# Expert logits computed as eight extra columns of a matrix product, and what has to be prepared for that earlier

## The chip, the cores and the metric

The kernel runs on one core of one Trainium2 chip. The metric is the device time of one execution in microseconds (us), the median of several runs. The core's engines run side by side and synchronise by semaphores: TensorE (PE, with its weight loads PEld), VectorE (DVE), ScalarE (ACT), GpSimd (POOL) and the DMA queue of SyncE (SP).

## The reference

```python
# 1. attention: r, k, v are (4, 8, 768, 48); a decayed state per head
for t in range(S):
    cur = einsum('bhd,bhe->bhde', u[None] * kt, vt)
    y[:, :, t] = einsum('bhd,bhde->bhe', rt, state + cur)
    state = w[None, :, :, None] * state + einsum('bhd,bhe->bhde', kt, vt)
x = y.transpose(0, 2, 1, 3).reshape(3072, 384)
# 2. feed-forward, d_ff = 2048
h = x @ w_in
g = h - np.tanh(h)
x2 = g @ w_out                      # (3072, 384)
# 3. eight experts, one for each token (d_ff = 1024)
xn = x2 / (norm(x2) + 1e-6); en = expert_emb / (norm(expert_emb) + 1e-6)
logits = xn @ en.T / tau            # (3072, 8)
expert = argmax(logits); gate = softmax(logits)[expert]
out = gate * (maximum(x2 @ w1[expert], 0) @ w2[expert])
```

## The kernel before

The kernel has three stages, each a block with its own program for every engine. A block ends when all engines have ended theirs.

**Attention** goes over `CH` = 6 chunks of 128 time steps, and in each over `B` = 4 batches: 24 tiles, numbered `n = B * c + b`. For a tile SP loads about 1.2 MB into one of four sets of buffers, once the tile four places earlier is done (`summed`, counted by PE's last transposes of a tile, L525, and two other semaphores). POOL multiplies r by k (L290) and by u (L292), ACT sums the product over each head in eight pieces (L339, the "bonus"), and POOL multiplies v by these sums (`bv`, L301). DVE scales r and k two tiles ahead (`rs` L376, `ks` L377, and k once more as `kst`, L384, for the state), masks the scores (`am`, L442), adds up the result (L433) and advances the state (`state_sum` L457, `state` L461). PE computes scores (L489), the state's update (L502), the product with the state (L509), the masked scores by v (L517), and the transposes of `bv` (L525). The first and the last chunk are written out by the program, the four between are a loop. A piece of 128x512 of the weights `w_in` (b = 0, 1) and `w_out` (b = 2, 3) comes with each tile. ACT rounds it to the high part (L332), POOL forms the low part (L295): all the feed-forward's products are made of three, high by high, high by low and low by high. After its last tile PE runs eight rounds of `keep_warm` (products of the identity by itself, two records each, L76).

**The feed-forward** takes 6 groups `g` of 512 tokens, and in each 16 blocks `f` of 128 hidden units. For a block PE makes 9 products of 512 columns (`first`), ACT `usq`, `tanh` and `quad`, DVE `diff`, `poly`, `large`, a second step of `poly` and a predicated copy (which count `h_used` and `g_done`), ACT the high part `g_h` and DVE the low part `g_l` of the result. `second(g, f)` multiplies it by `w_out`: 12 products of 384 columns, three for each of four tiles of 128 tokens, in four banks `y_ps`. It comes `LAG` = 3 blocks after `first`. `SPLIT` = blocks 9, 11 and 13 also hold the split of the next group's x (ACT, then DVE, L901). In each block one piece of the experts' weights is loaded by SP, split by ACT (L827) and POOL (L705) and stored again as `w12_h` and `w12_l`: 96 pieces in 96 blocks. POOL's split waits for `g_done` of its block.

For the logits PE turns each finished tile of 128 tokens (`turn_x2`, three transposes, L750) and multiplies it by the normed embeddings (`logit`, three products of eight columns, two records each, L758); ACT copies the turned tile between. Five groups do this within the next group's blocks (`TURN`), the last one at the end. There the order on ACT is four copies of `y_ps` and four sums of squares (`square_sum`, L840).

**The experts' stage** sorts tokens by expert and computes 31 tiles.

## Time and profile before

| | us |
|---|---|
| median of 3 runs (lowest, highest) | 932.28 (931.85, 932.81) |
| the profiled execution's own time | 932.17 |
| its span in the profile | 930.1 |
| granted TensorE clock, mean over the span | 0.98 |

The profile shows one execution. Busy times of engines overlap; a row of the timeline gives start, duration, engine, line and operands, and in brackets how long the engine had been idle and what ended that. Line numbers are those of the program above. A granted clock of 1.00 is 2.4 GHz, of 0.50 1.2 GHz.

### The profile page before, as it was taken

To read this page: it belongs to the slowest core of one execution; us is meant where nothing else is said; L and a number is where in the kernel's file an instruction comes from. 1 tells how busy PE (TensorE), PEld (TensorE's weight loads), DVE (VectorE), ACT (ScalarE), POOL (GpSimd) and SP (SyncE) were. 2 spreads that over 40 slices of the span, in tenths; PEclk is the share of its full clock that TensorE was granted. 3 is DMA by queue.
4 is the path that set the end of the run, shared out by engine and by line. 5 is a ranking of instruction groups with operands and counts; after the bars stand their busy time and mean duration, and the time that the engine had idled before them with its cause. 6 is when DMAs were issued, how large, how long until landed. Compare 5 with 4: busy or idle time off the path is not lost. (4 is left out here: it accounts for less than half of the span.)

```text
span 930.1 us, 18916 instructions
## 1 busy us (share of the span) xinstructions
PE 876.5 (94%) x5314; PEld 788.3 (85%) x5315; DVE 606.2 (65%) x991; ACT 477.4 (51%) x1225; POOL 349.1 (38%) x372
## 2 busy tenths in 40 slices
PE   4887778999999999999999999889999999999995
PEld 4776667799998998999999999879989999898994
DVE  8899998899889889889989988641121211212110
ACT  3455555677766766766767765313233333333331
POOL 9789995233323323323223322232222232222211
PEclk8899999999999999999999999889999999999998
DMA  7799885665755855755755654678857836811100
GB/s 223 193 256 258 249 249 138 198 201 185 262 168 185 256 169 175 259 175 170 249 174 183 209 181 158 242 257 297 317 210 266 304 110 241 311 40 34 47 6 1
DMA packets 106810, 181.46 MB, mean 195 GB/s; under 512 B 11051, under 2 KB 32717, under 8 KB 106768
## 3 DMA queue, kind: packets, MB, share of 16 engines
q1 hardware_dynamic: 92816, 165.40, 54.8%
q0 software_dynamic: 3968, 10.82, 3.5%
q10 hardware_dynamic: 9984, 4.72, 1.9%
q8 instruction: 21, 0.34, 0.2%
q14 instruction: 21, 0.17, 0.1%
HBM read 116.41 MB, written 65.86 MB: 196 GB/s over the span
## 5 line engine op out<-in xcount | busy, mean ns | idle before, releaser
L705 POOL TENSOR_TENSOR ew_l<-ew_raw,ew_h 128x512 fp32r<-128x512 f32 x96 | 128.2, 1335 | 299.9 <-DVE poly L927 297.0
L649 PE MATMUL y_ps<-wout_h,g_h 128*128 128x384 f32 x384 | 129.5, 337 | 1.1 <-DVE g_l L918 1.1
L651 PE MATMUL y_ps<-wout_h,g_l 128*128 128x384 f32 x384 | 129.3, 337 | 0.0
L650 PE MATMUL y_ps<-wout_l,g_h 128*128 128x384 f32 x384 | 129.1, 336 | 0.0
L1346 DVE TENSOR_TENSOR ex_hT_l<-e_bank,ex_hT_h 128x512 fp32r<-128x512 f32 x62 | 39.9, 686 | 127.4 <-ACT ex_hT_h L1496 127.4
L649 PE MATMUL h_ps<-xT_h,win_h 128*128 (+1 forms) x288 | 115.8, 402 | 2.1 <-DVE diff L908 2.1
L808 ACT ACTIVATE usq<-h_ps 128x512 f32<-128x512 f32 x96 | 55.9, 582 | 115.7 <-PE h_ps L651 102.9
L651 PE MATMUL h_ps<-xT_h,win_l 128*128 (+1 forms) x288 | 113.5, 394 | 0.0
L650 PE MATMUL h_ps<-xT_l,win_h 128*128 (+1 forms) x288 | 113.4, 394 | 0.0
L1373 POOL DMA_INDIRECT out_dram<-ex_o_sb,put_i x31 | 31.1, 1003 | 210.0 <-ACT ex_o_sb L1480 192.6
L1496 ACT ACTIVATE ex_hT_h<-e_bank 128x512 fp32r<-128x512 f32 x62 | 33.7, 596 | 122.3 <-PE e_bank L1406 118.2
L1338 DVE TENSOR_TENSOR ex_xT_l<-e_bank,ex_xT_h 128x384 fp32r<-128x384 f32 x31 | 17.3, 558 | 116.9 <-ACT ex_xT_h L1472 106.4
L1404 PE MATMUL e_bank<-w_h,ex_hT_h 128*128 x248 | 86.6, 349 | 1.3 <-ACT ex_o_sb L1480 1.3
L1406 PE MATMUL e_bank<-w_h,ex_hT_l 128*128 x248 | 84.1, 339 | 0.0
L1405 PE MATMUL e_bank<-w_l,ex_hT_h 128*128 x248 | 83.8, 338 | 0.0
L908 DVE TENSOR_TENSOR diff<-h_ps,tanh 128x512 f32<-128x512 f32 x96 | 66.1, 688 | 25.9 <-ACT tanh L809 25.4
L927 DVE COPY_PREDICATED poly<-large,diff 128x512 f32<-128x512 uint8 x96 | 71.7, 747 | 16.8 <-DVE poly L923 16.8
L1488 ACT ACTIVATE ex_hid<-e_bank 128x512 f32<-128x512 f32 x62 | 37.2, 599 | 79.5 <-PE e_bank L1406 79.5
L1404 PE MATMUL e_bank<-w_h,ex_xT_h 128*128 x186 | 76.0, 409 | 1.2 <-DVE ex_xT_l L1338 1.2
L649 PEld LDWEIGHTS y_ps<-wout_h,g_h 128*128 128x128 f32 x384 | 72.1, 188 | 5.7 <-issue 1.4
L650 PEld LDWEIGHTS y_ps<-wout_l,g_h 128*128 128x128 f32 x384 | 72.2, 188 | 4.2
L339 ACT ACTIVATE rku_out<-rku 128x48 f32<-128x48 f32 x192 | 43.7, 229 | 60.1 <-POOL rku L292 60.1
(206 smaller groups left out, 2126.2 us busy)
## 6 DMA issues: line engine op xcount, KB each, us to landing
ew_raw<-in_w SPq DMA_DIRECT2D x96, 256.0 KB, 3.1
w_h<-ew_h SPq DMA_DIRECT2D x96, 256.0 KB, 3.2
w_l<-ew_l SPq DMA_DIRECT2D x96, 256.0 KB, 2.0
w_h<-w_h SPq DMA_DIRECT2D x16, 1536.0 KB
w_l<-w_l SPq DMA_DIRECT2D x16, 1536.0 KB
rT_sb<-in_rT SPq DMA_DIRECT2D x48, 96.0 KB, 2.6
kT_sb<-in_kT SPq DMA_DIRECT2D x48, 96.0 KB, 2.8
k_sb<-in_k SPq DMA_DIRECT2D x24, 192.0 KB, 3.0
```

The costliest lines, as they stand in the source:

```text
L339: last_sum = act.activation(rku_out[:, head], rku[:, b % 2, head], ACT.Copy, accum_out=bonus[:, b % 2, h:h + 1])
L649: pe.matmul(out, lh, rh, start=start, stop=False)
L650: pe.matmul(out, lh, rl, start=False, stop=False)
L651: return pe.matmul(out, ll, rh, start=False, stop=stop)
L705: pool.tensor_tensor(ew_l[:, s, :], ew_raw[:, f % SPARE, :], ew_h[:, s, :].bitcast(F32), ALU.subtract).then_inc(ew_l_made, 1)
L808: act.activation(usq[:, :], h_ps[f % 2][:, :], ACT.Square).then_inc(u_done, 1)
L908: dve.tensor_tensor(diff[:, f % 2, :], h_ps[f % 2][:, :], tanh[:, f % 2, :], ALU.subtract).then_inc(h_used, 1)
L927: dve.copy_predicated(poly[:, f % RING, :], large[:, f % 2, :], diff[:, f % 2, :]).then_inc(g_done, 1)
L1346: dve.tensor_tensor(hT_l[:, hf, :], hT_ps[hf][:, :], hT_h[:, hf, :].bitcast(F32), ALU.subtract).then_inc(hT_split, 1)
L1404: pe.matmul(ps, lh, w_h[:, slot, cols], start=start, stop=False)
L1405: pe.matmul(ps, lh, w_l[:, slot, cols], start=False, stop=False)
L1406: return pe.matmul(ps, ll, w_h[:, slot, cols], start=False, stop=stop)
```

## The change

Since `logits = (g @ w_out) @ en.T` up to the norm, the eight logits of a token are also `g @ (w_out @ en.T)`. The kernel now makes `w_logit = w_out @ en.T` (2048x8), and each product of `second` has 392 columns instead of 384.

- PE's transposes, the logit products, ACT's and DVE's copies between them and the copy of the logits go away; ACT copies eight columns of `y_ps` for each tile of tokens.
- `w_logit` is made at attention's end: 48 products of eight columns on PE (`logit_weights`), after the last tile, and a copy on ACT. The embeddings are normed by DVE in the first chunk and turned in the last. For it `w_out` comes transposed in place of the pieces with b = 2, 3; these pieces are not split any more. `keep_warm` at the end has four rounds instead of eight.
- `w_out` itself is loaded and split in the feed-forward's first group, 16 pieces of 128x384, in the place of that group's experts' pieces. Groups 1 to 4 take 20 experts' pieces instead of 16, two of them in blocks 3, 7, 11 and 15; the last group takes 16.
- POOL's split waits for `g_done` in groups 1 to 5, not in the first.
- In attention's first chunk the state isn't read (it is zero) and not added to; in the last chunk it isn't advanced.
- `usq` has two buffers instead of one.

```diff
+                            sp.dma_start(raw[:, b, :], w_in[c, b]).then_inc(loaded[b], 16)
+                        else:
+                            sp.dma_start(piece_of(c, b, woT_flat), w_outT[c, b - 2]).then_inc(loaded[b], 16)
...
 
-                        wait_apart(pool, passed_low, (high_made, n + 1))
-                        pool.tensor_tensor(piece_of(c, b, (win_l, wout_l)), raw[:, b, :],
-                                           piece_of(c, b, (win_h, wout_h)).bitcast(F32),
-                                           ALU.subtract).then_inc(low_made, 1)
+                        if b < 2:
+                            wait_apart(pool, passed_low, (high_made, 2 * c + b + 1))
+                            pool.tensor_tensor(piece_of(c, b, win_l_flat), raw[:, b, :],
+                                               piece_of(c, b, win_h_flat).bitcast(F32),
...
                 take(CH - 1, B - 1)
                 store(CH - 1, B - 1)
+                act.wait_ge(wl_done, 1)
+                act.activation(w_logit[:, :, :].rearrange("p f e -> p (f e)"), upd[:, 0:KF * E],
+                               ACT.Copy).then_inc(wl_taken, 1)
 
...
-
+                            if not isinstance(c, int) or c + 1 < CH - 1:
+                                scale_t(c + 1, b + 2 - B)
+
+                        if is_first(c) and b == B - 1:
+                            scale_emb()
+                        if last and b == 0:
+                            dve.wait_ge(emb_turned, 1)
+                            dve.tensor_copy(embT[:, :, :], upd[:, 0:KD * E].rearrange("p (a e) -> p a e", a=KD)
+                                            ).then_inc(embT_made, 1)
+                        if last:
+                            continue
...
                         dve.wait_ge(updated, n + 1)
-                        wait(dve, state_new, n)
+                        if is_first(c):
+                            dve.tensor_tensor(padded(state[0:ROWS, b, :, :]), by_pair(upd[0:ROWS, 0:DM]),
+                                              wblock[0:ROWS, :, :, :], ALU.mult).then_inc(state_new, 1)
+                            continue
+                        dve.wait_ge(state_new, n)
                         dve.tensor_tensor(state_sum[0:ROWS, :, :, :], padded(state[0:ROWS, b, :, :]),
                                           by_pair(upd[0:ROWS, 0:DM]), ALU.add).then_inc(state_added, 1)
...
+                def turn_emb():
+                    pe.wait_ge(emb_scaled, 1)
+                    pe.wait_ge(state_new, NT - B)
+                    for a in range(KD):
+                        t = pe.transpose(upd[:, a * E:(a + 1) * E], emb_n[:, a * P:(a + 1) * P], ident[0:E, 0:E])
+                    t.then_inc(emb_turned, 1)
+
...
+                def logit_weights(blocks):
+                    pe.wait_ge(embT_made, 1)
+                    for b in range(2, B):
+                        pe.wait_ge(loaded[b], 16 * LOADS * CH)
+                    for f in blocks:
+                        for a in range(KD):
+                            last = pe.matmul(upd[:, f * E:(f + 1) * E], woT_sb[:, f, a, :], embT[:, a, :],
+                                             start=(a == 0), stop=(a == KD - 1), skip_group_check=True)
+                    return last
...
+                        pe.wait_ge(scaled_t, n + 1)
+                        if is_first(c) or b == 0:
+                            wait(pe, state_new, n)
+                        else:
+                            pe.wait_ge(state_added, n - B)
...
-                    last.then_inc(state_read, 1)
+                    if not is_first(c):
+                        wait(pe, state_new, n - B + 1)
+                        for q in range(PAIRS):
+                            last = pe.matmul(y[b % 2][0:ROWS, q * P:(q + 1) * P], state[0:ROWS, b, q, 0:ROWS],
+                                             rs[0:ROWS, b, q, :], start=(q == 0), stop=False, skip_group_check=True)
+                        last.then_inc(state_read, 1)
...
-def feed_forward(nc, x2_dram, x_sb, load_group, x_loaded, x_stored, emb_sb, emb_c, ident, embT,
-                 win_h, win_l, wout_h, wout_l, logits_raw, sumsq, small, tau, w12, w12_h, w12_l):
+                logit_weights(range(KF)).then_inc(wl_done, 1)
+                keep_warm(pe, banks[0], ident, 4)
...
-        def piece_of(x, g, f):
-
-            n = KF * g + f
+        def pieces(g, last):
+
+            return KF if last or (isinstance(g, int) and g == 0) else KF + EXTRA
+
+        def pieces_at(g, last, f):
+
+            if pieces(g, last) == KF:
+                return [f]
+            return [f + f // EXTRA] + ([f + f // EXTRA + 1] if f % EXTRA == EXTRA - 1 else [])
...
+                def load_piece(g, j):
+                    slot = j % SPARE
+                    if is_first(g):
+                        sp.dma_start(ew_raw[:, slot, 0:DM], w_out[j * P:(j + 1) * P, :]).then_inc(ew_loaded[slot], 16)
+                    else:
+                        sp.dma_start(ew_raw[:, slot, :], piece_of(w12, g, j)).then_inc(ew_loaded[slot], 16)
+
+                def store_piece(g, j):
+                    slot = j % MADE
+                    sp.wait_ge(ew_h_made, before(g) + j + 1)
+                    sp.dma_start(piece_of(w12_h, g, j), ew_h[:, slot, :].bitcast(F32)).then_inc(ew_h_stored[slot], 16)
+                    sp.wait_ge(ew_l_made, before(g) + j + 1)
+                    sp.dma_start(piece_of(w12_l, g, j), ew_l[:, slot, :].bitcast(F32)).then_inc(ew_l_stored[slot], 16)
 
...
+                        for j in pieces_at(g, last, f):
+                            if is_first(g):
+                                sp.wait_ge(ew_l_made, j + 1)
+                            else:
+                                store_piece(g, j)
+                            if j + SPARE < pieces(g, last):
+                                load_piece(g, j + SPARE)
+                            elif not last:
+                                load_piece(g + 1, j + SPARE - pieces(g, last))
...
-                def low(g, f):
-                    s = f % MADE
-                    wait_apart(pool, passed_pool, (g_done, KF * g + f + 1), (ew_h_made, KF * g + f + 1),
-                               (ew_l_stored[s], 16 * (KF // MADE * g + f // MADE)))
-                    pool.tensor_tensor(ew_l[:, s, :], ew_raw[:, f % SPARE, :], ew_h[:, s, :].bitcast(F32),
-                                       ALU.subtract).then_inc(ew_l_made, 1)
+                def low(g, j):
+                    slot = j % MADE
+                    raw = ew_raw[:, j % SPARE, :]
+                    if is_first(g):
+                        pool.wait_ge(ew_h_made, j + 1)
+                        pool.tensor_tensor(wout_l[:, j, 0:DM], raw[:, 0:DM], wout_h[:, j, 0:DM].bitcast(F32),
+                                           ALU.subtract).then_inc(ew_l_made, 1)
+                    else:
+                        wait_apart(pool, passed_pool, (ew_h_made, before(g) + j + 1),
+                                   (ew_l_stored[slot], 16 * (stores(g) + j // MADE + 1)))
+                        pool.tensor_tensor(ew_l[:, slot, :], raw, ew_h[:, slot, :].bitcast(F32),
+                                           ALU.subtract).then_inc(ew_l_made, 1)
 
                 def group(g, last):
                     for f in range(KF):
-                        low(g, f)
+                        if not is_first(g):
+                            wait_apart(pool, passed_pool, (g_done, KF * g + f + 1))
+                        for j in pieces_at(g, last, f):
...
                 def second(g, f):
                     pe.wait_ge(gh_done, KF * g + f + 1)
                     pe.wait_ge(gl_done, KF * g + f + 1)
+                    if is_first(g):
+                        pe.wait_ge(ew_l_made, f + 1)
+                        if f == 0:
+                            pe.wait_ge(wl_split, 1)
                     for b in range(B):
...
-                        last = products(pe, y_ps[b][:, 0:DM], g_h[:, f % RING, cols], g_l[:, f % RING, cols],
+                        last = products(pe, y_ps[b][:, 0:DL], g_h[:, f % RING, cols], g_l[:, f % RING, cols],
...
+                def piece_high(g, j):
+                    slot = j % MADE
+                    raw = ew_raw[:, j % SPARE, :]
+                    if is_first(g):
+                        act.wait_ge(ew_loaded[j % SPARE], 16 * (j // SPARE + 1))
+                        act.activation(wout_h[:, j, 0:DM], raw[:, 0:DM], ACT.Copy).then_inc(ew_h_made, 1)
+                    else:
+                        wait_apart(act, passed_x, (ew_loaded[j % SPARE], 16 * (uses(g, SPARE) + j // SPARE + 1)),
+                                   (ew_h_stored[slot], 16 * (stores(g) + j // MADE + 1)),
+                                   (ew_l_made, before(g) + j + 1 - MADE))
+                        act.activation(ew_h[:, slot, :], raw, ACT.Copy).then_inc(ew_h_made, 1)
...
                 def finish(g, b):
                     act.wait_ge(y_done, B * g + b + 1)
 
                     wait(act, x2_stored, 16 * B * g)
-                    wait(act, x2_turned, B * g)
                     wait(act, y_squared, B * g)
+                    act.activation(logits_of(g, b), y_ps[b][:, DM:DL].unsqueeze(1), ACT.Copy)
                     act.activation(x2_sb[:, b, :], y_ps[b][:, 0:DM], ACT.Copy).then_inc(y_copied, 1)
```

## Rows read from the trace of the kernel before

**Rows 1.** Stretches: length, busy us of each engine, granted clock, DMA share, GB/s.
```profile
57.00:143.71 86.71, 70.17 (x783) 60.06 (x781) 86.20 (x136) 44.14 (x270) 79.88 (x61) 0.98 0.89 252
...
171.70:583.40 411.70, 410.70 (x2153) 373.11 (x2152) 368.34 (x583) 290.71 (x572) 126.89 (x95) 1.00 0.61 197
```

**Rows 2.** Timeline of POOL in attention: start, us, idle before and releaser.
```profile
143.71 1.32 POOL L290 TENSOR_TENSOR rku<-r_sb,k_sb 128x384 f32<-128x384 f32 x1
145.10 1.00 POOL L292 TENSOR_TENSOR rku<-rku,u_sb 128x384 f32<-128x384 f32 x1
146.06 1.72 POOL L295 TENSOR_TENSOR wout_l<-raw,wout_h 128x512 fp32r<-128x512 f32 x1
148.13 1.42 POOL L301 TENSOR_TENSOR bv<-v_sb,bonus 128x384 f32<-128x384 f32 x1 [0.35 <-ACT rku_out L339]
149.51 1.32 POOL L290 TENSOR_TENSOR rku<-r_sb,k_sb 128x384 f32<-128x384 f32 x1
...
153.94 0.83 POOL L301 TENSOR_TENSOR bv<-v_sb,bonus 128x384 f32<-128x384 f32 x1 [0.80 <-ACT rku_out L339]
```

**Rows 3.** Timeline of DVE in attention.
```profile
146.58 1.75 DVE L377 TENSOR_TENSOR ks<-kT_sb,pk 112x512 f32<-112x512 f32 x1
```

**Rows 4.** Timeline of PE in attention's first chunk.
```profile
23.59 1.94 PE L509 MATMUL bank<-rs,state 112*112 112x128 f32 x8
```

**Rows 5.** Stretches in attention's first chunk, columns as in rows 1.
```profile
24.00:28.00 4.00, 4.00 (x44) 3.39 (x42) 3.42 (x9) 1.39 (x6) 0.09 (x1) 0.81 0.00 0
```

**Rows 6.** Timeline of PE in attention's last two tiles and at its end.
```profile
144.53 1.05 PE L509 MATMUL bank<-rs,state 112*112 112x128 f32 x8
...
155.82 0.65 PE L525 MATMUL bank<-ident,bv 128*112 128x128 f32 x4
156.31 2.52 PE L76 MATMUL bank<-ident 128*128 128x128 f32 x16
```

**Rows 7.** Timeline of PE in the feed-forward.
```profile
541.90 0.34 PE L651 MATMUL y_ps<-wout_h,g_l 128*128 128x384 f32 x1
542.08 0.73 PE L758 MATMUL t_ps<-embT,x2T 128*128 128x8 f32 x6
542.66 0.52 PE L750 MATMUL t_ps<-ident,x_sb 128*128 128x128 f32 x3
542.94 0.48 PE L649 MATMUL h_ps<-xT_h,win_h 128*128 128x512 f32 x1
543.25 0.39 PE L650 MATMUL h_ps<-xT_l,win_h 128*128 128x512 f32 x1
543.49 0.39 PE L651 MATMUL h_ps<-xT_h,win_l 128*128 128x512 f32 x1
```

**Rows 8.** Timeline of DVE in the feed-forward.
```profile
568.97 0.69 DVE L908 TENSOR_TENSOR diff<-h_ps,tanh 128x512 f32<-128x512 f32 x1 [0.18 <-ACT tanh L809]
...
570.77 0.68 DVE L918 TENSOR_TENSOR g_l<-poly,g_h 128x512 fp32r<-128x512 f32 x1
...
573.14 0.69 DVE L908 TENSOR_TENSOR diff<-h_ps,tanh 128x512 f32<-128x512 f32 x1 [0.17 <-ACT tanh L809]
```

**Rows 9.** Timeline of POOL in the feed-forward.
```profile
569.00 1.30 POOL L705 TENSOR_TENSOR ew_l<-ew_raw,ew_h 128x512 fp32r<-128x512 f32 x1 [3.56 <-DVE poly L927]
```

**Rows 10.** Timeline of DVE at the feed-forward's end.
```profile
582.13 1.23 DVE L918 TENSOR_TENSOR g_l<-poly,g_h 128x512 fp32r<-128x512 f32 x1 [0.81 <-ACT g_h L820]
...
589.97 0.19 DVE L964 COPY logits_raw<-y_ps 128x32 f32<-128x32 f32 x1 [0.93 <-PE y_ps L758]
```

**Rows 11.** Timeline of POOL at the feed-forward's end.
```profile
581.52 1.29 POOL L705 TENSOR_TENSOR ew_l<-ew_raw,ew_h 128x512 fp32r<-128x512 f32 x1 [2.86 <-DVE poly L927]
```

**Rows 12.** Timeline of PE at the feed-forward's end.
```profile
586.97 2.96 PE L758 MATMUL y_ps<-embT,x2T 128*128 128x8 f32 x24
```

**Rows 13.** Timeline of ACT at the feed-forward's end.
```profile
588.79 0.19 ACT L840 ACTIVATION_READ_ACCUMULATOR junk<-x_sb 128x1 f32 x1
```

**Rows 14.** Stretches after the feed-forward, columns as in rows 1.
```profile
592.00:594.00 2.00, 2.00 (x10) 1.83 (x9) 1.83 (x6) 0.00 (x0) 0.61 (x3) 0.54 0.92 296
```

More of the change, by code:

```diff
@@ new lines, in tile @@
+                def tile(c, b, final):
+                    n = B * c + b
+                    if not final:
+                        pe.wait_ge(scaled_t, n + 1)
[4 more added lines that the diff above has]
+                        for q in range(PAIRS):
+                            pair = slice(q * 2 * D, (q + 1) * 2 * D)
+                            last = pe.matmul(upd[0:ROWS, pair], kst[:, b % 2, q, :], v_sb[:, b, pair],
+                                             start=(q == 0), stop=True, skip_group_check=True)
+                        last.then_inc(updated, 1)
+                    elif b == 0:
+                        turn_emb()
+                    wait(pe, y_taken, n - 1)
+                    if not is_first(c):
+                        wait(pe, state_new, n - B + 1)
+                        for q in range(PAIRS):
+                            last = pe.matmul(y[b % 2][0:ROWS, q * P:(q + 1) * P], state[0:ROWS, b, q, 0:ROWS],
+                                             rs[0:ROWS, b, q, :], start=(q == 0), stop=False, skip_group_check=True)
+                        last.then_inc(state_read, 1)
@@ L533, in chunk, with feed_forward @@
                             score(c + 1, 0)
-                        tile(c, b)
+                        tile(c, b, last)
                 score(0, 0)
                 chunks(pe, chunk)
-                keep_warm(pe, banks[0], ident, 8)
-def feed_forward(nc, x2_dram, x_sb, load_group, x_loaded, x_stored, emb_sb, emb_c, ident, embT,
-                 win_h, win_l, wout_h, wout_l, logits_raw, sumsq, small, tau, w12, w12_h, w12_l):
+                logit_weights(range(KF)).then_inc(wl_done, 1)
+                keep_warm(pe, banks[0], ident, 4)
+def feed_forward(nc, x2_dram, x_sb, load_group, x_loaded, x_stored, ident, win_h, win_l, w_out, w_logit,
+                 logits_raw, sumsq, small, tau, w12, w12_h, w12_l):
     LAG = 3
@@ L545, in feed_forward @@
     SPARE = 4
-    TURNS = KF // SPARE
     MADE = 2
+    EXTRA = 4
+    DL = DM + E
     G = B * P
@@ L883, in _ @@
                     x_high(0, a)
+                act.activation(wout_h[:, :, DM:DL], w_logit[:, :, :], ACT.Copy).then_inc(wl_high, 1)
                 act.activation(junk[:, 0:1], bias[:, 0:1], ACT.Tanh)
@@ L910, in begin @@
                     dve.wait_ge(q_done, n + 1)
-                    dve.tensor_tensor(poly[:, f % RING, :], tanh[:, f % 2, :], usq[:, :],
+                    dve.tensor_tensor(poly[:, f % RING, :], tanh[:, f % 2, :], usq[f % 2][:, :],
                                       ALU.mult).then_inc(tu_done, 1)
-                    dve.tensor_scalar(large[:, f % 2, :], usq[:, :], SMALL, None,
+                    dve.tensor_scalar(large[:, f % 2, :], usq[f % 2][:, :], SMALL, None,
                                       ALU.is_gt).then_inc(large_done, 1)
@@ L1544 @@
         "w_in": by_piece(inputs["moe_w_in"]),
-        "w_out": by_piece(inputs["moe_w_out"]),
+        "w_out": np.ascontiguousarray(inputs["moe_w_out"]),
+        "w_outT": turned_pieces(inputs["moe_w_out"]),
         "emb": np.ascontiguousarray(inputs["moe2_expert_emb"]),
```

235 lines of the change are left out of this document (88 added, 147 removed).

## The prediction

> **What bounds the kernel now.** I read the stretches first, to see which engine is never idle in which stage, then the timelines at the seams. In attention, from 57 to 143.71 us, DVE is busy 86.20 of 86.71 us and POOL 79.88, and the DMA engines have a share of 0.89 [rows 1]. In the feed-forward PE is busy all the time but 1 us, and DVE has 368.34 of 411.70 us, 89% [rows 1]. So PE's instructions there count one for one, and DVE stands 11% behind it: the reader should keep that distance in mind.
>
> In attention one tile takes 149.51 - 143.71 = 5.80 us [rows 2], and nobody waits long. Two engines hold each other up. POOL's split takes 1.72 us in that tile; DVE's `ks` starts during it, takes 1.75 us and ends 0.55 us after the split [rows 2, 3]. `bv` takes 1.42 us beside a busy DVE, 0.83 us for the last tile, when DVE has less to do [rows 2]. An operation of DVE with both inputs in SBUF and one of POOL seem to exclude each other.
>
> In the feed-forward the same pair meets only once. A block's period on DVE is 573.14 - 568.97 = 4.17 us, of which 0.18 us is a wait for ACT's `tanh`, so DVE alone needs 3.99 [rows 8]. POOL's split starts at 569.00, as `g_done` comes, and ends at 570.30, before `g_l` at 570.77: it lies beside `diff`, `poly` and `large`, which read PSUM, and `g_l` takes 0.68 us [rows 8, 9]. Only at the end does a split, 581.52 to 582.81, overlap `g_l`, which then takes 1.23 us and ends 0.55 us after it [rows 10, 11], as `ks` did.
>
> **The change part by part.** The sum is made against the profiled execution's 932.2 us: its span of 930.1 and 2.1 around it. The median of the runs is 0.1 us from that, so the same sum holds for it.
>
> *Logits inside the feed-forward.* The six records of a tile's logits go from 542.08 to 542.66 and the three transposes to 542.94, 0.86 us; the next product's spacing is 543.25 - 542.94 = 0.31 instead of 0.24, some 0.08 more [rows 7]. That is 0.94 us for a tile, on a PE without idle time, and 5 groups of 4 tiles have it: 20 x 0.94 = 18.8 us less.
>
> *Eight more columns.* Products of 384 columns start 0.18 us apart and of 512 columns 0.24 [rows 7], so a column costs 0.06/128 us = 0.47 ns. 6 x 16 x 12 = 1152 products of `second` x 8 columns x 0.47 ns = 4.3 us more. Below: none, if the start is set by the weight load of another product; above: 0.18 x 8/384 = 3.8 ns each, 4.3 as well. I take 4.3.
>
> *The end of the feed-forward.* Its last tiles' transposes and logits, to DVE's copy at 589.97 + 0.19 = 590.16, go away [rows 10]. But ACT's last sum of squares ends at 588.79 + 0.19 = 588.98 [rows 13] and four copies of eight columns come before it, about 0.2 us each, as DVE's small copy of 0.19 [rows 10]: 589.8. Gain 0.3 us (0 to 1.2).
>
> *Attention.* Twelve splits of `w_out` leave POOL, and twelve roundings ACT, which waits for POOL anyway. Without the split the chain POOL, bonus on ACT, `bv` stays: the bonus ends where `bv` starts, 148.13, so POOL can't run ahead. What goes is the blocking. From 5.80 us per tile the floor is some 5.0: POOL's two products, 1.00 us each when nothing blocks them, ACT's sums from 146.10 to 148.13, `bv` 0.83, and the gaps between [rows 2]. DVE's own operations still block POOL's, above all `state`, which comes as `bv` does. I take half the distance, 0.4 us, for the six light tiles between tile 8 and tile 19: 2.4 us. Bounds: 0, if the DMA engines, at 0.89 and up to now 252 GB/s [rows 1], become the pacer, and 6 x 0.8 = 4.8. In the last chunk DVE also loses `kst`, `state_sum` and `state`: four tiles at 5.0 to 5.1 give 3 us. In the first chunk PE's product with the empty state goes, 1.94 us at the low clock [rows 4]; the DMA engines stand still from 24 to 28 us [rows 5] until PE has ended its first tile and the next loads may start. I take 1.0 of it, since the products behind it would then run before the clock rises. Last, PE's final transposes now follow DVE's `am` and end at 156.47 [rows 6]; afterwards they follow `bv`, which would end at about 148.9, since tile 23 starts 5.6 us or so earlier and is shorter by 0.3. With 0.9 us for PE that is 149.7: 6.8 us earlier, with the terms before in it (bounds 3 and 9).
>
> *Making `w_logit`.* 48 products of eight columns, two records each, 96 records, and PE has nothing to hide them behind: DVE, ACT and the stores of the last tile are done in 2 to 3 us, and every engine waits for the block's end. In the feed-forward six such records take 0.58 us, 0.097 each [rows 7]; at its end 24 take 2.96 us with a wait in it, 0.123 each [rows 12]. So 9.3 to 11.8 us; I take 0.11, between the two, 10.5 us. `keep_warm` falls from 2.52 [rows 6] to 1.26 us. PE's end moves from 156.31 + 2.52 = 158.83 to 149.7 + 10.5 + 1.3 = 161.5: 2.7 us later, and the feed-forward's start with it. ACT's copy runs beside `keep_warm`. Without the change in attention the same would have cost 9.5 us.
>
> The Trainium skill, page "TensorE: Matmul & The Clock Gate", section "LDWEIGHTS (loading the stationary operand)", gives a weight load as its columns divided by 1.2 GHz, an estimate of 107 ns for 128 columns. By it the 96 records would take 10.2 us, and the sum would be 0.3 us lower; the trace's rows lie on both sides of it.
>
> *Where POOL's splits now fall.* In group 0 they follow ACT's copy instead of `g_done`: that copy ends shortly before `g_l` starts, so a split of 384 columns (1.0 us) runs into `g_l`. By 1.23 - 0.68 = 0.55 us at most, by my phases 0.4, each block of DVE gets longer: 3.99 + 0.4 = 4.39 us against PE's new 4.17 + 12 x 0.0037 = 4.21. PE is then paced by DVE: 16 x 0.18 = 2.9 us. In groups 1 to 4 the second split of a block starts at `g_done` + 1.35 and ends at + 2.65, while `g_l` would start at + 1.85: `g_l` ends 0.75 us later, four times in a group, 3.0 us. Together with the three splits of x (0.6 each) DVE needs 16 x 3.99 + 1.8 + 3.0 = 68.6 us for a group, PE 67.4: 1.2 us each, 4.8 in all. The bounds are 0, since `second` runs three blocks behind and can swallow some 4 us, and 2.9 + 4.8 = 7.7. At the start that cover is empty, PE already waits for DVE there; later it fills slowly. I take 4.5 us. The second buffer of `usq` frees ACT in the first blocks, but DVE is the one that is late there: nothing. DMA traffic rises by a quarter in groups 1 to 4 from a share of 0.61 [rows 1]: hidden. The small loads at the block's start are shorter (192 instead of 256 KB), which lets DVE begin about 0.3 us earlier.
>
> The Trainium skill, page "SBUF — State Buffer", section "Who interferes with whom", says that a VectorE instruction with two SBUF inputs and a GpSimd instruction that reads SBUF block each other for the whole instruction. The `ks` of 1.75 us agrees. Read as it stands it speaks against this change, since it sends the second split against `g_l`; with it in full the sum would be 3.2 us higher, by the undisturbed `g_l` rows 4.5 us lower.
>
> **The sum:** 932.2 - 18.8 + 4.3 - 0.3 + 2.7 + 4.5 - 0.3 = 924.3 us.
>
> **The rivals.** *The clock falls.* From 592 to 594 us the granted clock is 0.54 [rows 14], and before it lie 24 products of eight columns [rows 12]. If such products don't hold the clock at 2.4 GHz, the 96 records end at 1.2 GHz, and the feed-forward starts at it. The product with the state takes 1.94 us at the low clock against 1.05 at the high one [rows 4, 6], so half of the records doubled, 5 us, is the upper bound and 1 us the lower; I take 3. Nine products of 512 columns at twice their 0.24 us would cost 2.2 more, of which I take 1, since DVE has its own start to make: 928.3. Against it: between the products of the states and scores PE is idle for part of each tile too, and the clock in attention is 0.98 [rows 1].
>
> *PE stays the only bound of the feed-forward*, the lock is swallowed by the three blocks of lag: 924.3 - 4.5 = 919.8. For it speaks that PE today never waits for DVE after the first blocks; against it DVE's 89% [rows 1].
>
> *DVE becomes the pacer in earnest, and the kernel is slower.* If the double pieces shift POOL and ACT so that each split meets `g_l` (0.55 us), a block takes 3.99 + 0.55 + 0.11 for x = 4.65 us instead of 4.21. For 80 blocks that is 35 us: 924.3 - 4.5 + 35 = 955. It decides from 12.4/80 = 0.155 us per block above 4.21, that is 4.37. Against it: the wait for `g_done` puts the first split of a block beside `diff` each time.
>
> *The light tiles bring nothing*, because the DMA engines pace attention, and only the last chunk gains: 924.3 + 2.4 + 1.0 = 927.7.
>
> **How the numbers follow.** The forecast has 0.4, the clock's fall 0.25, PE alone 0.15, attention without gain 0.12, the slower case 0.04, combinations at the upper end 0.04. The likeliest case's own range is 921 to 927.5. The whole range takes in PE alone with a little more from attention, 918.5, and the clock's fall with 2 us of lock more, 930.5; it leaves the slower case out. A change within 0.2% (1.9 us) can hardly be told from none with this kernel's runs. Faster by more (below 930.4) 0.89, within 0.06, slower 0.05.
>
> **What would show it.** The page: L750 and L758 gone, 96 records of the new product of eight columns within 9 to 12 us between the last transposes and `keep_warm`, granted clock 1.00 in that stretch and behind it. The feed-forward's products of 392 columns 3 to 4 ns further apart. `g_l` with a mean of 0.75 to 0.9 us instead of 0.68, and waits of PE for `h_used` or `g_l` of some 4 us beyond today's. Tiles without a split at 5.4 us beside 5.8. The forecast is wrong if PE waits for DVE in every block, if the clock is 0.5 at the feed-forward's start, or if attention's tiles keep 5.80 us.

## The result, and the profile after

The kernel after takes 936.51 us, the median of 6 runs (934.41 to 937.90), and the kernel before 932.58 on the same chip (6 runs, 931.85 to 934.17): a ratio of 1.0037 with an interval of 1.0021 to 1.0053. It is slower, by some 4 us, where 924.3 had been forecast. The profiled execution took 934.41 us with a span of 932.7, so it is 2.2 us longer than the profiled one of before, and 2.6 us by the spans. Here and below the ratios leave out executions that took over 1.5% more than the fastest of their kernel: one of `e8_wide`, two of `e11_early_fixed` and one of `e12_fixed_made4_gate`.

The stretches of the kernel after, from attention through the seam to the feed-forward (length, busy us of PE, PE's loads, DVE, ACT, POOL, granted clock, DMA share, GB/s):

```profile
57.00:143.71 86.71, 74.47 (x828) 63.06 (x825) 85.08 (x141) 42.50 (x279) 65.64 (x56) 0.98 0.88 260
150.00:154.00 4.00, 4.00 (x39) 4.00 (x37) 0.69 (x1) 0.60 (x1) 0.00 (x0) 1.00 0.38 100
154.00:156.00 2.00, 2.00 (x15) 2.00 (x14) 0.00 (x0) 0.00 (x0) 0.00 (x0) 0.68 0.01 4
156.00:170.00 14.00, 13.52 (x63) 13.25 (x64) 0.06 (x1) 0.84 (x3) 0.00 (x0) 0.50 0.00 0
170.00:172.00 2.00, 2.00 (x10) 1.86 (x10) 1.79 (x3) 1.98 (x5) 0.00 (x0) 0.55 0.70 210
...
178.00:589.00 411.00, 401.01 (x1988) 362.44 (x1987) 383.11 (x587) 297.58 (x589) 141.96 (x111) 1.00 0.62 207
```

Two things are new beside [rows 1]. From within the stretch 154 to 156 us into that of 170 to 172 the granted clock stands at its lower level, 1.2 GHz, though PE is never idle until `keep_warm` is over. And in the feed-forward PE is idle for 10 us of 411 where it had been for 1, while the busy share of DVE has gone from 89% to 93%. POOL is relieved in attention, 65.64 us for 79.88.

PE's timeline over the seam, which answers to [rows 6]:

```profile
149.94 0.65 PE L595 MATMUL bank<-ident,bv 128*112 128x128 f32 x4
150.43 16.58 PE L553 MATMUL bank<-embT,woT_sb 128*128 128x8 f32 x96
166.86 2.05 PE L76 MATMUL bank<-ident 128*128 128x128 f32 x8
169.39 2.04 PE L76 MATMUL y_ps<-ident 128*128 128x128 f32 x8 [0.48 <-PEq L234]
171.09 0.77 PE L734 MATMUL h_ps<-xT_h,win_h 128*128 128x512 f32 x1
```

Attention's last transposes end at 150.59, 5.9 us earlier than before. Then the 96 records take 16.58 us, and the feed-forward starts at 171.09 instead of 160.88. Its last product ends at 589.98, 418.9 us after its first one started; before it was 424.95. From there to the experts' first product it is 32.3 us against 33.5, and the experts' part has nearly the same length in both (310.4 us, before 310.8). The four differences, 10.2 - 6.1 - 1.2 - 0.4, make up the 2.6 us by which the span grew, up to rounding.

### The profile page after: what moved, and what is told of

Its sections match the earlier page's. It is cut to its first block and busy times, and to the rows that moved or that the text cites. A ratio compares the mean times of both kernels' runs of the same rounds, so it can differ in the third digit from the quotient of the medians.

```text
span 932.7 us, 18741 instructions
## 1 busy us (share of the span) xinstructions
PE 871.7 (93%) x5122; PEld 782.4 (84%) x5123; DVE 604.2 (65%) x973; ACT 476.2 (51%) x1230; POOL 337.3 (36%) x376
## 5 line engine op out<-in xcount | busy, mean ns | idle before, releaser
L734 PE MATMUL y_ps<-wout_h,g_h 128*128 128x392 f32 x384 | 132.9, 346 | 8.4 <-ACT x_sb L912 7.4
L735 PE MATMUL y_ps<-wout_l,g_h 128*128 128x392 f32 x384 | 131.2, 342 | 0.0
L736 PE MATMUL y_ps<-wout_h,g_l 128*128 128x392 f32 x384 | 131.0, 341 | 0.0
L734 PE MATMUL h_ps<-xT_h,win_h 128*128 (+1 forms) x288 | 113.3, 393 | 2.0 <-DVE diff L973 2.0
L892 ACT ACTIVATE g_h<-poly 128x512 fp32r<-128x512 f32 x96 | 60.9, 634 | 60.8 <-DVE poly L992 60.4
L904 ACT ACTIVATE ew_h<-ew_raw 128x512 fp32r<-128x512 f32 x96 | 60.7, 633 | 38.6 <-DMA w_h<-ew_h 28.3
L983 DVE TENSOR_TENSOR g_l<-poly,g_h 128x512 fp32r<-128x512 f32 x96 | 77.5, 808 | 0.8 <-ACT g_h L892 0.8
```

The lines of the kernel that those rows point to most:

```text
L734: pe.matmul(out, lh, rh, start=start, stop=False)
L735: pe.matmul(out, lh, rl, start=False, stop=False)
L736: return pe.matmul(out, ll, rh, start=False, stop=stop)
L892: act.activation(g_h[:, f % RING, :], poly[:, f % RING, :], ACT.Copy).then_inc(gh_done, 1)
L904: act.activation(ew_h[:, slot, :], raw, ACT.Copy).then_inc(ew_h_made, 1)
L983: dve.tensor_tensor(g_l[:, f % RING, :], poly[:, f % RING, :], g_h[:, f % RING, :].bitcast(F32), ALU.subtract).then_inc(gl_done, 1)
```

## The experiments

A run is compared with the kernel after by the difference of the two ratios to the kernel before. Lengths are from one profiled execution each. "Start" is the feed-forward's first product, "length" the time from there to the end of its last one. Five runs leave the feed-forward as it is in the kernel after (418.9 us): their lengths are 417.6 (`e1_spread`), 421.0 (`e3_wide_between`), 418.5 (`e7_early`), 420.4 (`e8_wide`) and 419.3 (`e11_early_fixed`). So a difference of 2 us in length says little, one of 4 us a lot.

**The burst, spread over the last chunk.** `e1_spread` puts 13 of the 16 blocks into the last chunk's tiles:

```diff
+                EARLY = [range(0, 5), range(5, 9), range(9, 13)]
                 def tile(c, b, final):
...
+                    if final and b > 0:
+                        logit_weights(EARLY[b - 1], CH - 1)
                     pe.wait_ge(masked, 2 * n + 2)
...
-                logit_weights(range(KF)).then_inc(wl_done, 1)
+                logit_weights(range(13, KF)).then_inc(wl_done, 1)
```

> The changed kernel with 13 of the 16 blocks of the products for w_logit moved into attention's last three tiles, 3 blocks left behind them. Theory A (the 96 records behind the last tile lie on the path, at 1.2 GHz for most of their 16.6 us): the first product of the feed-forward starts at 158 to 162 us instead of 171.1, and the time falls by 9 to 13 us, to 924 to 928. Theory B (the time is lost inside the feed-forward, whose start doesn't matter much because VectorE is late there anyway): less than 3 us, 934 or more. Theory C (the tiles have no room for 78 records either, and each gets 2 us longer): 929 to 931.

Measured 937.46 us, ratio to before 1.0035 (1.0019 to 1.005): the gain of the first theory isn't there. The time is in the second theory's range, but not for its reason, since the feed-forward starts at 177.5, 6.4 us later than in the kernel after. Its PE timeline:

```profile
145.99 3.41 PE L553 MATMUL bank<-embT,woT_sb 128*128 128x8 f32 x30
...
151.46 2.08 PE L535 MATMUL bank<-rs,ks 48*128 48x128 f32 x16
153.47 2.05 PE L580 MATMUL bank<-rs,state 112*112 112x128 f32 x8
155.31 5.13 PE L553 MATMUL bank<-embT,woT_sb 128*128 128x8 f32 x24
```

The first 30 records still run at 1.00 (144 to 150 us). Behind them the clock falls (0.52 from 150 to 156), and now attention's own products run at the low clock too: the state product takes 2.05 us at 153.47, where it takes 1.13 at 145.03. The gain from hiding the burst was paid back in the tiles.

**The burst alone.** `e2_before_burst` is the kernel before with 96 such records behind attention, computing nothing of use:

```diff
                 chunks(pe, chunk)
-                keep_warm(pe, banks[0], ident, 8)
+                for f in range(3 * KF):
+                    pe.matmul(banks[0][:, f * E:(f + 1) * E], ident[:, :], ident[:, 0:E], start=True, stop=True,
+                              skip_group_check=True)
+                keep_warm(pe, banks[0], ident, 4)
```

> The kernel before with 48 products of eight columns (96 records, to a bank that nobody reads) behind attention's last tile, and four rounds of keep_warm instead of eight: only the burst, alone. Theory A with the clock's fall: 96 records take 15 to 17 us and the time rises by 14 to 17 us to 947 to 950. If such a burst alone held the clock at 2.4 GHz (0.1 us a record): plus 8 to 9 us, 941. If it were hidden: 932.5.

Measured 952.4 us, ratio 1.0191 (1.017 to 1.0212): 18 us more. Its PE timeline:

```profile
159.98 17.70 PE L539 MATMUL bank<-ident 128*128 128x8 f32 x96
177.53 2.05 PE L76 MATMUL bank<-ident 128*128 128x128 f32 x8
```

and the stretch in the middle of it, with the granted clock at 0.50:

```profile
164.00:175.00 11.00, 11.00 (x54) 11.00 (x53) 0.00 (x0) 0.00 (x0) 0.00 (x0) 0.50 0.01 1
```

So the cost needs neither the lighter last chunk nor the feed-forward's new form. The 96 records take 0.18 us each here too.

**Wide products in between.** `e3_wide_between` adds one product of 512 columns behind each six records of the burst:

```diff
                                              start=(a == 0), stop=(a == KD - 1), skip_group_check=True)
+                        pe.matmul(banks[0][:, :], win_h[:, 0, 0:P], win_h[:, 1, 0:512], start=True, stop=True)
```

> The changed kernel with a product of 512 columns (0.24 us at 2.4 GHz, its result unused) behind each of the 16 blocks of six records, 3.8 us of work more. If the clock falls because eight-column products pass too little through TensorE, it stays up: 16 x (0.58 + 0.24) = 13.1 us instead of 16.6, granted clock 1.00, and the time falls by 3 to 6 us. If the clock falls for another reason, the stretch takes 16.6 + 7 = 23 us and the time rises by 4 to 7 us.

Measured 946.22 us, ratio 1.0128 (1.01 to 1.0155), 8 to 9 us above the kernel after. PE's timeline in it:

```profile
153.15 0.73 PE L553 MATMUL bank<-embT,woT_sb 128*128 128x8 f32 x6
153.74 0.47 PE L555 MATMUL bank<-win_h 128*128 128x512 f32 x1
154.05 1.09 PE L553 MATMUL bank<-embT,woT_sb 128*128 128x8 f32 x6
155.00 0.77 PE L555 MATMUL bank<-win_h 128*128 128x512 f32 x1
```

The clock falls at 154 us all the same: the records' six go from 0.73 to 1.09 and then to 1.28 us. Wide products for a third of the time did not hold it, and the whole stretch, 151.35 to 176.05, takes 24.7 us, near the 23 of the second case.

**The same weights, made wide.** `e8_wide` swaps the operands: `embT` is stationary, `w_out`'s transpose streams in 512 columns, and the [8, 2048] result is turned afterwards.

```diff
+                    for i in range(4):
+                        for a in range(KD):
+                            last = pe.matmul(scores[i // 2][i % 2][0:E, :], embT[:, a, :], woT_sb[:, 4 * i:4 * i + 4, a, :],
+                                             start=(a == 0), stop=(a == KD - 1))
+                        last.then_inc(wide_done, 1)
+                    pe.wait_ge(wide_copied, 4)
+                    for f in range(KF):
+                        last = pe.transpose(upd[:, f * E:(f + 1) * E], ks_flat[0:E, f * P:(f + 1) * P],
+                                            ident[0:E, 0:E])
```

> The kernel after, with the same weights of the logits made in the same place but wide: the embedding is the stationary operand (8 columns of weights) and w_out's transpose the moving one, 12 products of 512 columns into four banks, four copies by VectorE, then 16 turns of 8 x 128. Nothing is left out. Theory A (it is the small size of the products behind attention, not TensorE being busy, that lets the granted clock fall): the 12 products take about 0.85 to 0.9 us each at 2.4 GHz, 10 to 11 us, the 16 turns 1.6 to 3 us, the first product of the feed-forward starts near 166 to 168 where it was 171.1, and the time falls by 3 to 6 us. Theory B (the clock falls for another reason, such as the end of attention's load on TensorE as a whole): the 512-column products show 1.7 us each and the time rises by 8 or more.

Measured 934.78 us, ratio 1.0005 (0.9991 to 1.0019), 3 us below the kernel after by the ratios. PE's timeline, and below it the stretch of the 24 records:

```profile
154.13 10.47 PE L562 MATMUL bank<-woT_sb,embT 128*8 128x512 f32 x24
165.38 1.15 PE L567 MATMUL bank<-ident,ks 8*128 8x8 f32 x16 [0.77 <-DVE ks L521]
...
170.22 0.54 PE L748 MATMUL h_ps<-xT_h,win_h 128*128 128x512 f32 x1
```

```profile
154.13:164.60 10.47, 10.47 (x25) 2.08 (x24) 2.72 (x4) 0.60 (x1) 0.00 (x0) 1.00 0.15 39
```

This settles that the form of the products matters. PE is busy without a gap in both kernels, and in the same place. With 96 records of eight columns the clock falls, with 24 of 512 columns it stays at 2.4 GHz for all of the 10.47 us. Two things differ between them, the columns that stream through and the weights that are loaded (128 columns for each narrow record, 8 for each wide one), and no run separates these. From attention's last transpose to the start it is 16.0 us here and 20.5 in the kernel after. The start was expected at 166 to 168 and came at 170.2, since attention's last transposes ended at 154.2 in this profile, 3.6 us later than in the kernel after.

**A few records per tile.** `e7_early` turns `emb` in the first chunk and makes one block in each of three tiles of the chunks 1 to 4 and four in the last chunk. TensorE's chunks are written out.

```diff
+                        if not is_first(c) and b > 0:
+                            logit_block(c, (c - 1) * 3 + b - 1)
...
-                logit_weights(range(KF)).then_inc(wl_done, 1)
```

> The kernel after, with the products of w_logit made one block of weights (3 eight-column products, 6 records) at a time in the tiles of the chunks 1 to 4, and the last four blocks in the last chunk, so that no run of 96 records stands behind attention; TensorE's chunks are written out and not looped. Nothing is left out. Theory A (a dense run of eight-column products lets the granted clock fall to 1.2 GHz; 6 records in a tile, between 384-column score and state products, do not): the clock stays at 2.4 GHz from attention's last tiles on, the last transposes end at about 151, the first product of the feed-forward starts at 153 to 156 where it was 171.1, and the time falls by 14 to 17 us against the kernel after, to about 920 to 923. Theory B (any eight-column product in attention lets the clock fall, as in the last chunk's tiles before): the tiles themselves slow, POOL's period is passed, and the time stays within 4 us of the kernel after. Theory C (the late start of the feed-forward is given back later, since VectorE paces the groups anyway): start earlier by 16 but time lower by less than 8.

Measured 942.29 us, ratio 1.0089 (1.0072 to 1.0106). All three theories missed, since I had built in a wait. (The expectation also calls the tiles' products 384 columns wide; a record of them has 96 to 128.) PE's timeline in the last chunk:

```profile
159.19 1.42 PE L553 MATMUL bank<-embT,woT_sb 128*128 128x8 f32 x6 [6.73 <-DMA woT_sb<-in_w_outT]
```

The block waited for pieces of its own chunk, and behind it stood the state and attention products that the next loads wait for; after the 6.73 us of idle time PE ran at 1.2 GHz. Attention ended at 177.5.

`e11_early_fixed` takes only pieces of the chunk before:

```diff
+                WHEN = [[[], [], [], []], [[], [], [0], [1]], [[], [2], [3], [4]], [[], [5], [6], [7]],
+                        [[], [8], [9], []], [[10, 11], [12], [13], [14, 15]]]
```

> As e7_early, but no block of the logits' weights is made before its pieces have been in for a chunk: tiles of the chunks 1 to 4 take blocks 0 to 9 and wait only for loads of the chunk before, the last chunk takes 10 to 15 (two, one, one and two in its four tiles). Nothing is left out. In e7_early TensorE waited for the transposed pieces of its own chunk, 6.73 us at one place, and attention's last transposes ended at 177.5. Theory A (that wait alone cost e7_early its gain; 6 to 12 records in a tile leave the clock up): the last transposes end at 149 to 154 and the first product of the feed-forward starts at 154 to 158, time 14 us below the kernel after, 919 to 923. Theory B (eight-column products between the tiles' products slow attention as such): the last transposes end above 160 and the time stays above 930.

Measured 926.91 us, ratio 0.9918 (0.989 to 0.9945), 1.2% below the kernel after's ratio, 11 us, and above the 919 to 923 expected. PE's timeline:

```profile
138.11 1.50 PE L553 MATMUL bank<-embT,woT_sb 128*128 128x8 f32 x12 [0.48 <-DVE state L508]
...
140.75 1.95 PE L597 MATMUL bank<-am,v_sb 128*48 128x128 f32 x16
...
144.75 0.83 PE L553 MATMUL bank<-embT,woT_sb 128*128 128x8 f32 x6
...
156.18 1.06 PE L76 MATMUL bank<-ident 128*128 128x128 f32 x8
...
160.43 0.61 PE L745 MATMUL h_ps<-xT_h,win_h 128*128 128x512 f32 x1
```

The start is at 160.4, 10.7 us earlier than in the kernel after and 2 to 6 later than expected. Attention's last transposes end at 156.35, 5 to 7 us later than in the profiles without records in the tiles (149.2 to 151.5, leaving out `e8_wide`'s 154.2); no run shows how much of that the records cost. A stretch of 4.7 us in the last chunk, behind idle time and twelve records, had a mean clock of 0.64; a stretch at the low clock is there without records in `e8_wide` (0.58 from 139 to 143, am's products 1.95 us at 140.06), so records aren't needed for it.

**Two buffers or four.** `e4_made4` only sets `MADE = 4`.

> The changed kernel with four buffers instead of two (MADE = 4) for the split experts' pieces on their way to memory. Theory R (two pieces in one block meet a ring of two, ScalarE waits 38 us for stores and splits, its tanh and its copies of y_ps come late, and TensorE waits 7.4 us for them): ScalarE's waits for w_h<-ew_h and for POOL go, TensorE's wait for x_sb goes, and the time falls by 3 to 8 us. Theory L (the feed-forward is longer than its products because POOL's second split blocks VectorE's g_l): the time changes by less than 1.5 us and g_l's mean stays at 0.81 us.

Measured 933.84 us, ratio 0.9996 (0.9972 to 1.0021), 3.8 us below the kernel after. The waits in the feed-forward of the kernel after:

```profile
ACT ew_h L904 <- DMA w_h<-ew_h: 28.3, 38, 1.7
...
ACT ew_h L904 <- POOL ew_l L806: 10.0, 16, 1.2
...
PE y_ps L734 <- ACT x_sb L912: 7.4, 5, 2.0
```

The first two are gone in `e4_made4`, the third falls to 4.2 us where it was expected to go, and the length falls from 418.9 to 414.2 us. All of it is in the groups 1 to 4, where PE's products of y begin 68.1 us after those of the group before, each time, instead of 68.5 to 70.3. With two pieces in one block, ACT comes to the second while the stores of the last ones still read the buffers. `g_h`, `usq` and the copies of y stand behind it on ACT, and PE waits for the copies.

**Group 0.** `e5_gate0` holds POOL's split in the first group behind `g_done` (the expectation says `g_l`; what is counted is the predicated copy, and the split then runs beside the next operations):

```diff
-                        if not is_first(g):
-                            wait_apart(pool, passed_pool, (g_done, KF * g + f + 1))
+                        wait_apart(pool, passed_pool, (g_done, KF * g + f + 1))
```

> The kernel after, with one wait more: in group 0 POOL's split of an output-weight piece waits for VectorE's g_l of its block, as it does in the later groups. Nothing is left out. Theory A (the free-running split holds the shared port and stretches VectorE's operations, blocks of 4.24 us where they were 3.9): the blocks of group 0 fall to 3.9 to 4.0, the group by 3 to 5 us, and the time by 3 to 5. Theory B (the split is on the chain itself, its result is what TensorE's second products wait for): TensorE waits for wout_l in group 0, the blocks stay at 4.2 or grow, time within 1.5 us or up.

Measured 931.37 us, ratio 0.9989 (0.9967 to 1.0012), 4 to 5 us below the kernel after. DVE and then POOL in group 0 of the kernel after:

```profile
193.27 1.04 DVE L983 TENSOR_TENSOR g_l<-poly,g_h 128x512 fp32r<-128x512 f32 x1
```

```profile
192.75 1.02 POOL L801 TENSOR_TENSOR wout_l<-ew_raw,wout_h 128x384 fp32r<-128x384 f32 x1 [3.23 <-ACT wout_h L899]
```

and in `e5_gate0`:

```profile
195.75 0.68 DVE L982 TENSOR_TENSOR g_l<-poly,g_h 128x512 fp32r<-128x512 f32 x1
```

```profile
194.24 1.02 POOL L801 TENSOR_TENSOR wout_l<-ew_raw,wout_h 128x384 fp32r<-128x384 f32 x1 [2.87 <-DVE poly L991]
```

The split ends at 193.77 and `g_l` 0.54 us later; with the wait, it falls beside `diff`, `poly` and `large`, which read PSUM and keep their 0.68 us. DVE's block goes from 4.24 to 3.88 us and its group 0 from 67.65 to 63.32. PE can't follow all of it, since its own work for a block takes 4.20: from its first product of y in group 0 to that of group 1 it is 67.1 us instead of 70.6. The length falls to 413.8.

**The eight columns.** `e13_narrow` leaves the logits' columns out of the second products, 384 in place of 392, and copies other columns into `logits_raw`.

> The kernel after, but the products of the second feed-forward step have 384 columns as before and the logits are left out (the first eight columns of y are copied in their place), to price the eight columns alone; their weights are still made behind attention. Theory A (TensorE sets the pace of most blocks, so each column counts, as the prediction's 4.3 us had it): the feed-forward is 414 to 415 us where it was 418.9, and the time 4 us lower. Theory B (VectorE with its stretched operations, and the waits for the halves' buffers, set the pace): under 1.5 us.

Measured 936.74 us, ratio 1.0046 (1.0029 to 1.0063): within the noise of the kernel after, length 419.8 us. The logits are wrong here, so tokens go to other experts, but from the feed-forward's end on the profile is as long as the kernel after's (342.5 and 342.7 us). In the kernel after the columns cost nothing that could be measured, although PE's products of y start 0.176 us apart here and 0.180 there (means over 250 to 296 us): the spacing is as predicted, the path isn't PE's.

**All of it.** `e10_early_made4_gate` joins `e7_early`, `e4_made4` and `e5_gate0`:

> The kernel after with all three: the logit weights made early in attention, four buffers in place of two for the expert weights' halves, and POOL's split of group 0 held behind g_l. Nothing is left out. If the three costs are separate they add up: 14 to 17 for the clock, 3 to 4 for the buffers, 3 to 5 for group 0: 911 to 917, a ratio of 0.975 to 0.984 to the kernel before. If VectorE's pace absorbs one into another: 917 to 922.

Measured 931.05 us, ratio 0.9977 (0.9957 to 0.9997). The late attention of `e7_early` (173.0 us) hides it, but the length is 410.0: the two repairs save 8.9 us together, 4.7 and 5.1 alone. The expected 911 to 917 us is missed for `e7_early`'s wait.

`e12_fixed_made4_gate` has `e11_early_fixed` in its place:

> e11_early_fixed with four buffers for the expert weights' halves and with POOL's split of group 0 held behind g_l. Nothing is left out. Its feed-forward should be as long as in e10_early_made4_gate, 410.0 us, and begin where that of e11_early_fixed does: 8 to 9 us below e11_early_fixed, 910 to 914, a ratio to the kernel before of 0.975 to 0.981. Rival: if attention ends as late as in e7_early, it stays at 931.

Measured 915.83 us (6 runs, 910.29 to 926.64), ratio 0.9811 (0.978 to 0.9842): 18 us faster than the kernel before and 21 than the one after, by the ratios, and 2 us above the 910 to 914 expected. Its profile caught the longest execution, 926.64, with a granted clock of 0.52 from 147 to 154 us and the start at 171.5; the length is 410.4. That stretch isn't all: before it the transposes of tile 19 already end at 144.4, in `e11_early_fixed` at 135.2, and the clock is 0.66 from 70 to 80 us. With `e11_early_fixed`'s start of 160.4 this profile would come to 915.6 us, near the median; so the executions probably differ in attention, but only this one was profiled, and what makes attention uneven stays open. What is left of the extra pieces shows in DVE's timeline in it:

```profile
321.69 0.68 DVE L993 TENSOR_TENSOR g_l<-poly,g_h 128x512 fp32r<-128x512 f32 x1
...
325.58 1.79 DVE L993 TENSOR_TENSOR g_l<-poly,g_h 128x512 fp32r<-128x512 f32 x1
```

and POOL's:

```profile
324.26 2.56 POOL L817 TENSOR_TENSOR ew_l<-ew_raw,ew_h 128x512 fp32r<-128x512 f32 x2 [2.90 <-DVE poly L1002]
```

A block with two splits keeps `g_l` until 327.37, 0.55 us behind the second split's end at 326.82, and is 4.98 us long instead of 3.88.

## Why the prediction was wrong

**The step that failed is "Making `w_logit`".** It priced the burst at 0.11 us a record, 10.5 us, from rows at the high clock; it measured 16.4 to the start of `keep_warm`, and `keep_warm` 2.05 for 1.3. With attention's end at 150.4 for 149.7 that puts PE's end at 168.9 where 161.5 was forecast, and the start 10.2 us later than before instead of 2.7. This is 7.5 of the 10.5 us by which the profile misses the sum's -7.9 (measured: +2.6 on the span); the feed-forward's length has 4.2, and what follows it gave back 1.3. `e2_before_burst` shows the burst's price by itself, `e8_wide` that it hangs on the form of the products, and `e11_early_fixed` what the kernel gains without it: 11 us, with the start at 160.4. The forecast had named this as a sign of being wrong: the clock is 0.55 at the feed-forward's start.

**The rival had the mechanism and not its price.** "The clock falls" got 0.25 and 4 us, 928.3. It took 3 us for the burst, between 1 and 5 for half the records doubled, and 1 for the feed-forward's start. In the trace the clock is full until 154 us, into which 36 of the records fit at 0.097 each; the other 60 took 12.9 us, 0.21 each. The burst was 5.9 us longer than priced, and `keep_warm`, which the rival left out, 0.75. [Rows 14] had the warning: 0.54 two us behind 24 such records. I held against it attention's mean clock of 0.98, but attention's products have 96 to 128 columns, so those rows said nothing about eight. A bound with all records doubled would have been 96 x 2 x 0.097 = 18.6 us, and the range would have reached 932; the measured 936.5 lies beyond that too, for the second miss.

**The second miss is the feed-forward**: 424.95 to 418.9 us, -6.1, where the steps gave -18.8 + 4.3 + 4.5 - 0.3 = -10.3, a length of 414.65. `e4_made4`, without the waits for buffers, has 414.2. So the extra pieces' way back to memory, which was put at nothing ("hidden"), is the miss, and the other terms add up to what was measured. That they do is partly luck, as their parts show:

- *The logits and transposes gone, -18.8.* PE's work did fall, but the time by less. By the mean distances of PE's products in `e12_fixed_made4_gate`, 12 x 0.178 + 9 x 0.228 = 4.19 us a block, PE needs 67.0 us for a group; with both repairs a group takes 68.1 from group 2 on, from one `diff` of a block 0 to the next on DVE, and in the kernel after groups 1 to 4 take 69.0 on average. Before it was 70.7. So 2.6 of the 3.8 us a group come in there, because DVE then sets the pace. The forecast had this limit, 68.6 us for DVE, in the term of 4.5.
- *Eight columns, +4.3.* The spacing was right, the sum wrong: nothing (`e13_narrow`). That DVE and ACT set the pace instead is what the gains of `e5_gate0` and `e4_made4` say. Counting the columns together with a slower DVE was counting twice. Whether they stay free once both repairs are in was not run.
- *Group 0 locked, 2.9 of it.* The mechanism was right; blocks of 4.24 for 4.39, and an undisturbed block of 3.88 for 3.99, as the kernel before has it in its own group 0. PE's group 0 shows a worth of 3.4 us (70.6 to 67.1), near the forecast; the length, of one profile, fell by 5.1.
- *Double pieces, +0.75 each.* Right in kind, low in size: 1.1 (1.79 - 0.68), since the two splits follow each other without a gap and `g_l` waits for both. In block 11, which also splits x, it is 0.57 (`g_l` of 1.25).
- *The small loads, -0.3.* Not shown: PE's first product of y comes 11.1 us behind the start before, and 10.2 to 11.4 behind it in the profiles with the new loads.
- *The buffers, put at nothing.* Missed. I followed the extra pieces through POOL and the DMA engines' share, and did not ask when the two buffers that ACT fills come free: 38 waits, 28.3 us on ACT, worth 4.7 us of the length.

The Trainium skill, page "SBUF — State Buffer", section "Who interferes with whom", spoke against the change with an exclusive lock between VectorE, reading two inputs from SBUF, and a GpSimd that reads SBUF. The traces agree: `g_l` of 1.04 and of 1.79 us, each ending 0.54 to 0.55 behind POOL's split.

**Attention was about right.** POOL's timeline in the kernel after, start of a tile with a split and without one:

```profile
68.01 1.31 POOL L307 TENSOR_TENSOR rku<-r_sb,k_sb 128x384 f32<-128x384 f32 x1
...
73.81 1.31 POOL L307 TENSOR_TENSOR rku<-r_sb,k_sb 128x384 f32<-128x384 f32 x1
...
79.02 1.32 POOL L307 TENSOR_TENSOR rku<-r_sb,k_sb 128x384 f32<-128x384 f32 x1
```

With the split 5.80 us, without it 5.21, where 5.4 was forecast. The end came 5.9 us earlier for 6.8; in four further profiles of the same attention (`e3_wide_between`, `e4_made4`, `e5_gate0`, `e13_narrow`) it came between 149.2 and 151.5, in `e8_wide` at 154.2. The first chunk brought hardly anything for the 1.0. What lies between the feed-forward's last product and the experts' first shrank by 1.2 us and not 0.3, the bound named.

So PE as the only bound and attention without gain are both refuted. The slower case I had named, `g_l` stretched by a split in every block and 955 us, is not what made it slower: in groups 1 to 4, 53 of 64 blocks have a `g_l` of 0.67 to 0.71 us.

## What to carry to other kernels

Price a long run of eight-column products on TensorE with most of it at the low clock, and what stands behind it too. If the same result can be had with the small operand stationary and the long one streaming (3 us here), or a few products at a time between the products of other work (11 us here), try that first. Place such products by the loads that they need and not by free time alone. When pieces of work are doubled up in one period, walk each ring that they pass (its buffers, the stores that free them, the engine that waits) before you look at bandwidth. When an engine is relieved by more than its distance to the second, the relief is worth that distance, and small costs added to the relieved engine can vanish, as the eight columns did here.

## What the runs showed of the hardware

- The granted clock fell to 1.2 GHz with TensorE busy without a gap: 96 records of eight columns, 16.58 us (0.17 each) against 0.097 in [rows 7]. The Trainium skill, page "TensorE: Matmul & The Clock Gate", section "What's actually happening", ties a low clock to an idle array; here the measurement decides against reading "busy" as "an instruction is always running".
- Six records and then a product of 512 columns, again and again, did not hold it either: 0.73 us for the six became 1.28. 24 records of 512 columns back to back did for their 10.47 us, at 0.436 us each.
- Two splits of GpSimd without a gap between them hold VectorE off for both: one instruction of 0.68 us took 1.79.
